# Attention and gated MLP on one core: attention scores from three products of split operands, and the steps around them put in another order

## The reference, cut to what matters

```python
B, H, S, D = 4, 8, 576, 64                      # fp32 throughout
scores = q @ k.T / 8 + bias[h, i, j]            # bias: a two-layer MLP of log distances
attn = softmax(scores)                          # row maximum subtracted, sum + 1e-9
x = (attn @ v), heads side by side              # 2304 tokens x 512
out = (sigmoid(x @ w_gate) * (x @ w_val)) @ w_out    # 512 -> 1536 -> 512
```

## Time and profile before

| | |
|---|---|
| median of three runs | 822.9 us (821.3 to 824.1) |
| the profiled execution: its own time / its span | 825.04 us / 823.2 us |
| mean granted TensorE clock over the span | 0.987 |
| busy: PE, DVE, ACT, POOL | 95%, 40%, 41%, 24% |
| bias stage | 0 to 79.2 us |
| attention stage | 79.2 to 361 us |
| MLP stage | 361 to 823 us |

### The profile page before, as it was taken

The page is one execution under the profiler, slowest core; times in us unless marked ns, Lnnn a source line. Parts: engine busy times, 40 slices in busy tenths (PEclk is TensorE's granted clock), DMA queues, the critical chain, the costliest instruction groups (busy, mean ns, idle before and its releaser), DMA issues.

```text
span 823.2 us, 13263 instructions
## 1 busy us (share of the span) xinstructions
PE 782.6 (95%) x5008; PEld 627.8 (76%) x5008; DVE 332.0 (40%) x797; ACT 338.0 (41%) x683; POOL 194.9 (24%) x362
## 2 busy tenths in 40 slices
PE   5684999999999999999989999999999999999998
PEld 2232666666666666669978998999899889989996
DVE  5894766666666666633320221123022202211220
ACT  5794666666666666643321221122022212212210
POOL 0000666646545545668400000000000000000000
PEclk9998999999999999999989999999999999999999
DMA  6684233242242233213322000100010010000001
GB/s 157 167 204 129 57 102 84 72 106 62 67 121 60 66 85 84 62 55 98 115 76 77 1 1 14 64 1 1 27 52 1 14 64 1 1 26 14 1 2 38
DMA packets 89152, 49.91 MB, mean 61 GB/s; under 512 B 60928, under 2 KB 80512, under 8 KB 89088
## 3 DMA queue, kind: packets, MB, share of 16 engines
q1 hardware_dynamic: 89088, 49.06, 21.9%
HBM read 28.98 MB, written 9.44 MB: 47 GB/s over the span
## 4 chain that ended last, share of the span: by engine, by line
PE 84%; DMA 5%; DVE 3%; ACT 3%; POOL 2%; SPq 1%; issue 1%; POOLq 0%; DVEq 0%; ACTq 0%
PE f_ps L950 18%; PE g_ps L900 15%; PE u_ps L900 15%; PE v_ps L882 10%; PE so_ps L816 9%; PE ty_ps L829 4%; PE tx_ps L841 3%; PE so_ps L811 2%; DVE feats L656 2%; DMA w_raw<-in_w_gate 2%; DMA x_raw<-in_w_out 2%; PE so_ps L764 2%; POOL w L480 1%; DMA bias<-bias_rows 1%; ACT feats L524 1%
## 5 line engine op out<-in xcount | busy, mean ns | idle before, releaser
L559 ACT ACTIVATE probs<-neg_scores,neg_max 128x576 f32<-128x576 f32 x144 | 110.6, 770 | 93.0 <-DVE neg_max L671 93.0
L900 PE MATMUL g_ps<-x_h,w 128*128 128x384 f32 x576 | 146.6, 335 | 1.2 <-DVE hid L733 1.2
L900 PE MATMUL u_ps<-x_h,w 128*128 128x384 f32 x576 | 146.3, 334 | 0.0
L733 DVE TENSOR_TENSOR hid<-u_ps,sig 128x384 f32<-128x384 f32 x72 | 40.1, 557 | 244.7 <-PE u_ps L900 244.7
L671 DVE CUSTOM_DVE_ANT_0 neg_scores<-so_ps,bias 128x576 f32<-128x576 f32 x144 | 104.0, 756 | 75.8 <-PE so_ps L816 54.6
L463 POOL TENSOR_SCALAR probs<-probs,recip 128x512 f32<-128x512 f32 x128 | 89.0, 695 | 187.6 <-DVE recip L685 187.6
L900 PEld LDWEIGHTS g_ps<-x_h,w 128*128 128x128 f32 x576 | 103.9, 188 | 2.3 <-DVE hid L733 1.6
L900 PEld LDWEIGHTS u_ps<-x_h,w 128*128 128x128 f32 x576 | 103.9, 188 | 0.5 <-issue 0.5
L620 ACT ACTIVATE h_h<-hid 128x384 fp32r<-128x384 f32 x72 | 37.9, 527 | 149.0 <-DVE hid L733 149.0
L900 PE MATMUL g_ps<-x_l,w 128*128 128x384 f32 x288 | 96.3, 334 | 0.0
L900 PE MATMUL u_ps<-x_l,w 128*128 128x384 f32 x288 | 96.2, 334 | 0.0
(11 more groups left out here) (68 smaller groups left out, 989.3 us busy)
## 6 DMA issues: line engine op xcount, KB each, us to landing
bias<-bias_rows SPq DMA_DIRECT2D x64, 144.0 KB
x_raw<-attn_transposed SPq DMA_DIRECT2D x6, 768.0 KB, 4.6
out<-out_sb SPq DMA_DIRECT2D x18, 256.0 KB, 2.0
q_raw<-in_q SPq DMA_DIRECT2D x32, 128.0 KB, 2.6
k_raw<-in_k SPq DMA_DIRECT2D x32, 128.0 KB, 2.5
v_main<-in_v SPq DMA_DIRECT2D x32, 128.0 KB, 2.3
w_raw<-in_w_gate SPq DMA_DIRECT2D x12, 256.0 KB, 2.9
w_raw<-in_w_val SPq DMA_DIRECT2D x12, 256.0 KB, 2.9
```

What stands on the lines that cost most here:

```text
L559: nc.scalar.activation(probs[s % RING][:, place, :], neg_scores[s % 2][:, place, :], ACT.Exp, bias=neg_max[:, stat(s, place)], scale=-1.0, ...
L733: nc.vector.tensor_tensor(hid[f % 2][:, :], u_ps[f % 3][:, 0:CH], sig[f % 2][:, :], ALU.mult).then_inc(gated, 1)
L900: last = nc.tensor.matmul(bank[f % 3][:, 0:CH], w[:, f, part, i, t, :], x[:, t, :], start=m == 0, stop=m == len(terms) - 1)
```

## The change

Scores are no longer fp32 products. q and k are held as a high part (float32r, written by ScalarE) and a low part (the difference, float32r, written by VectorE), and each score is the sum of three float32r products: high by high, low by high, high by low. The row tiles stay. Step 4's scores lie in the other two banks.

q is transposed two pairs ahead, in step 4 (the second pair's in the bias stage, at unit 18); k stays one pair ahead, in step 1, now ahead of the values. The values of a pair are computed wholly during the next one: three key tiles, two, three, two, in steps 0 to 3. Group 0 is copied out by VectorE, group 1 by ScalarE. In the steps with two places ScalarE does place 0's exponential behind `move_a`. There is one tile for the shifted scores instead of two. The drain holds three gate sums, one of them a step earlier.

```diff
-        EARLY_GATES = {STEPS: 0, STEPS + 1: 1}
+        EARLY_GATES = {STEPS - 1: 0, STEPS: 1, STEPS + 1: 2}
-        VALUE_SLOTS = {4: (0, 0, (0, 1)), 0: (1, 0, (2, 3)), 1: (1, 0, (4,)), 2: (1, 1, (0, 1, 2)), 3: (1, 1, (3, 4))}
+        VALUE_SLOTS = {0: (0, (0, 1, 2)), 1: (0, (3, 4)), 2: (1, (0, 1, 2)), 3: (1, (3, 4))}
...
+            def high_q(pair):
+                act.wait_ge(q_turned, pair + 1)
+                if pair >= 2:
+                    act.wait_ge(scored, SPP * (pair - 1) - 1)
+                nc.scalar.activation(qk_h[pair % 2][:, Q_MAIN:], q_turned_ps(pair), ACT.Copy).then_inc(q_high, 1)
...
-                if m == 1 and pair >= 1:
-                    copy_values(pair - 1, 0)
                 if m == 4 and pair >= 1:
-                    copy_values(pair - 1, 1)
-                for u, place in units:
+                    copy_values(pair - 1)
+                if m == 4 and pair + 2 < PAIRS:
+                    high_q(pair + 2)
+                if m == 1 and pair + 1 < PAIRS:
+                    high_k(pair + 1)
+                for u, place in units[:1]:
                     exponentials(s, u, place)
                 if 0 <= s - LAG < STEPS:
                     move_a(s - LAG)
                 if m == 0 and pair + 1 < PAIRS:
-                    copy_tails(pair + 1)
-                if m == 1 and pair + 1 < PAIRS:
-                    copy_q(pair + 1)
+                    high_tails(pair + 1)
+                for u, place in units[1:]:
+                    exponentials(s, u, place)
...
+            def low_q(pair):
+                dve.wait_ge(q_high, pair + 1)
+                nc.vector.tensor_tensor(qk_l[pair % 2][:, Q_MAIN:], q_turned_ps(pair), plain(qk_h[pair % 2][:, Q_MAIN:]),
+                                        ALU.subtract).then_inc(q_low, 1)
...
+                if m == 4 and pair + 2 < PAIRS:
+                    low_q(pair + 2)
+                if m == 1 and pair + 1 < PAIRS:
+                    low_k(pair + 1)
                 if 0 <= s - LAG < STEPS and (s - LAG) % SPP != R:
                     move_b(s - LAG)
-                if m == 1 and pair + 1 < PAIRS:
-                    copy_k(pair + 1)
+                if m == 1 and pair >= 1:
+                    copy_values(pair - 1)
+                if m == 0 and pair + 1 < PAIRS:
+                    low_tails(pair + 1)
...
             def turn_q(pair):
                 pe.wait_ge(q_in, 16 * Q_DMAS * (pair + 1))
-                if pair >= 2:
-                    pe.wait_ge(x_ready, 2 * (pair - 2) + 1)
+                if pair >= 3:
+                    pe.wait_ge(x_ready[1], pair - 2)
...
+                terms = ((high, high), (high, low), (low, high))
...
+                    for n, (qq, kk) in enumerate(terms):
...
+                        for place in (1, 0):
+                            rows = slice(place * D, (place + 1) * D)
+                            last = nc.tensor.matmul(score_ps(s, place)[:, a, :],
+                                                    qq[rows, Q_MAIN + m * P:Q_MAIN + (m + 1) * P], kk[rows, keys],
+                                                    start=n == 0, stop=n == len(terms) - 1)
...
+                if m == 1 and pair + 1 < PAIRS:
+                    turn_k(pair + 1)
+                if m == 1 and pair >= 1:
+                    values(pair - 1, *VALUE_SLOTS[m])
+                if m == 4 and pair + 2 < PAIRS:
+                    turn_q(pair + 2)
```

More of the change, by code:

```diff
@@ L31 @@
 PREP_UNIT = 6
+SECOND_UNIT = 18
 PAIRS = B * H // 2
@@ L114, in program @@
         valued = sem("valued")
-        x_ready = sem("x_ready")
+        x_ready = [sem(f"x_ready{i}") for i in range(2)]
         x_stored = [sem(f"x_stored{i}") for i in range(2)]
@@ L242, in bias_ps, with score_ps, q_turned_ps @@
             return so_ps[:, 2 * i:2 * i + 2, 0:HALF]
-        def score_ps(place):
-            return so_ps[:, 2 * place:2 * place + 2, 0:HALF]
+        def score_ps(s, place):
+            at = 2 if s % SPP == R else 2 * place
+            return so_ps[:, at:at + 2, 0:HALF]
+        def q_turned_ps(pair):
+            return tx_ps[:, 0:NT * P] if pair == 1 else v_ps[:, 0:NT * P]
         def set_rows(j):
@@ L394, in _ @@
                     load_k(pair + 2)
+                if m == 0 and 1 <= pair < PAIRS - 2:
                     sp.wait_ge(q_turned, pair + 2)
@@ L800, in scores @@
                 pair, m = divmod(s, SPP)
-                tile = qk[pair % 2]
+                high, low = qk_h[pair % 2], qk_l[pair % 2]
+                terms = ((high, high), (high, low), (low, high))
                 if m == 0:
-                    pe.wait_ge(k_copied, pair + 1)
-                    pe.wait_ge(tails_copied, pair + 1)
-                    pe.wait_ge(q_copied, pair + 1)
+                    pe.wait_ge(k_low, pair + 1)
+                    pe.wait_ge(tails_low, pair + 1)
+                    pe.wait_ge(q_low, pair + 1)
                 if s >= 1:
@@ L809, in scores @@
                     keys = slice(a * HALF, (a + 1) * HALF)
-                    if m == R:
-                        last = nc.tensor.matmul(score_ps(0)[:, a, :], tile[:, Q_TAIL:Q_MAIN], tile[:, keys],
-                                                start=True, stop=True)
-                        continue
-                    for place in (1, 0):
-                        rows = slice(place * D, (place + 1) * D)
-                        last = nc.tensor.matmul(score_ps(place)[:, a, :],
-                                                tile[rows, Q_MAIN + m * P:Q_MAIN + (m + 1) * P], tile[rows, keys],
-                                                start=True, stop=True)
+                    for n, (qq, kk) in enumerate(terms):
+                        if m == R:
+                            last = nc.tensor.matmul(score_ps(s, 0)[:, a, :], qq[:, Q_TAIL:Q_MAIN], kk[:, keys],
+                                                    start=n == 0, stop=n == len(terms) - 1)
+                            continue
+                        for place in (1, 0):
+                            rows = slice(place * D, (place + 1) * D)
+                            last = nc.tensor.matmul(score_ps(s, place)[:, a, :],
+                                                    qq[rows, Q_MAIN + m * P:Q_MAIN + (m + 1) * P], kk[rows, keys],
+                                                    start=n == 0, stop=n == len(terms) - 1)
                 last.then_inc(scored, 1)
@@ L891, in gate_part @@
                 if n == 0 and i == 0:
+                    pe.wait_ge(shifted, ALL - 1)
+                if n == 2 and i == 0:
                     pe.wait_ge(shifted, ALL)
@@ L909, in _ @@
                     turn_k(0)
+                if u == SECOND_UNIT:
+                    turn_q(1)
                 bias_unit(u)
@@ L913, in _ @@
                 pair, m = divmod(s, SPP)
-                back, group, tiles = VALUE_SLOTS[m]
-                of, c = pair - back, s - LAG
+                c = s - LAG
                 if s < STEPS:
                     scores(s)
-                if m == 1 and of >= 0:
-                    values(of, group, tiles)
+                if m == 1 and pair + 1 < PAIRS:
[4 more added lines that the diff above has]
+                    turn_q(pair + 2)
                 tails_of = pair + 1 if m == 0 and pair + 1 < PAIRS else None
@@ L927, in _ @@
                     turn_tails(tails_of)
-                if m == 1 and pair + 1 < PAIRS:
-                    turn_k(pair + 1)
-                    turn_q(pair + 1)
-                if m != 1 and of >= 0:
-                    values(of, group, tiles)
+                if m in (0, 2, 3) and pair >= 1:
+                    values(pair - 1, *VALUE_SLOTS[m])
                 if s in EARLY_GATES:
```

118 lines of the change are left out of this document (70 added, 48 removed).

## The result

| | before | after |
|---|---|---|
| median (20 runs each) | 822.0 us (820.2 to 824.1) | 825.4 us (823.8 to 829.8) |
| ratio of after to before | | 1.0047, 95% interval 1.0036 to 1.0057 |
| profiled execution: own time / span | 825.04 / 823.2 us | 825.99 / 824.2 us |

The change makes the kernel 0.5% slower. The time lies in the forecast range, 1.7 us above the forecast. The forecast gave the largest chance, 0.48, to no change that can be told; what came is a change that can just be told, and slower by over 0.3% had the chance 0.30.

A forecast was written before the change was run, and what follows sets the result against it. TensorE was taken to bound the kernel at 17.73 us a pair. Terms +1.7 + 0.6 - 1.8 - 1.1 - 0.3 + 1.7 = +0.8 on the median 822.9 gave 823.7 us, range 817 to 830.

The forecast's parts named there:

- The scores: TensorE's scores: two heads cost 1.00 us instead of 1.17, with a float32r product every 0.134; 0.85 saved a pair.
- The rival with bare loads: Row tiles' weight loads not hidden: 0.225 instead of 0.134 us a product, kernel 850 us or more; chance 0.04.
- The turn: ScalarE and VectorE from shift to shift: 3.36 us instead of 2.78, with `move_a` between the two exponentials.
- Both waits: TensorE waits 0.44 us ahead of `turn_q` in step 4 and 0.25 ahead of step 0's `transpose_b`.
- TensorE keeps the pace: Rival: TensorE alone sets a pair at 16.88 us, kernel 814.4; chance 0.22 for this or near it.
- 13 pairs: Steady attention pairs: 17.6 us a pair instead of 17.73, in all -1.8 us.
- wait for `x_half`: Step 4: TensorE's `turn_q` waits 0.44 us for ScalarE's copy of group 1.
- Pair 14: From step 1 of pair 14 to that of pair 15: 16.4 us instead of 17.5, so -1.1.
- The start: Bias stage, up to the first shift: +1.7 us, bounds 0 to 3.1.
- Unit 7: Bias stage: low parts of q, tails and k, with VectorE waiting on ScalarE's high parts, cost 1.15 us there.
- a low part of 0.69 at unit 18: Bias stage: VectorE's low part at unit 18 adds 0.69 us to the start.
- The weight line: Serial weight loads and splits behind the attention: start 10.8 us after the last step 4, +1.7; length stays 55.42.

The follow-up runs named there:

- e3: Kernel after, with VectorE's low part of q behind `move_b` in step 4 instead of ahead of it: ratio to before 1.0017, 823.3 us.
- e2: Kernel after, with both exponentials of a step ahead of `move_a` on ScalarE again: ratio to before 0.9977, 820.6 us.
- e10: Kernel e8, with `turn_q` behind `transpose_b` in step 4 on TensorE: ratio to before 0.9838, 809.3 us.
- e7: Kernel before, with the split float32r products added in its old order: ratio to before 1.0002, 822.5 us.
- e5: Kernel after, with the second pair's q handled at the bias stage's end and pair 2's q loaded in step 0 of pair 0: ratio to before 1.0026.
- e4: Kernel after, with weight loads issued ahead of the last pair's stores, two before each group: ratio to before 0.9996, 821.9 us.
- e6: Kernel after, each score one fp32 product of the high parts, low parts still made: ratio to before 1.0111, 831.3 us.
- e9: Kernel after, with two early gate sums in the drain instead of three: ratio to before 1.0042, 826.4 us.
- e11: Kernel after, with the second part of w_out split one f later: ratio to before 1.0066, 828.6 us.
- e1: Kernel after, with pair 2's q loads moved from the bias stage's store queue to step 0 of the attention: ratio to before 1.0045, 825.9 us.
- e8: Kernel after, with the edits of e2, e3, e4 and e5 together: ratio to before 0.9855, 810.1 us.

## Why the prediction was right, and where it was not

**The scores: right.** 0.98 for 1.00, and 0.133 for 0.134 from product to product. The rival with bare loads falls with it. The Trainium skill, page "TensorE: Matmul & The Clock Gate", section "The mechanism", lists overlap of a weight load with running matmuls only for another row group. Here all six products of a head have the same, and those of step 4, over the whole array, do too; both come every 0.133, so the loads stay hidden in float32r: the trace disagrees with that line. Another sentence of the same section also allows a load ahead where it goes to the background weight buffer, and that fits.

**The turn: right, to 0.1 at each mark.** Both waits stand where they were foreseen. e3 takes the second away, and e2 with e10 the first, so their causes are shown. Each handoff between engines had a row, and adding up rows from engine to engine held. TensorE's own sum was right as well: 16.88 by the rows, 16.87 in after less its waits, and 16.87 in e7. "TensorE keeps the pace" was the first rival. No run makes it quite true: e10, the nearest, has 17.02, with 0.17 of waiting left. Its ratio is 0.0209 below that of after (17 us), the edits at both ends included.

**13 pairs: -1.1 for -1.8**, a pair of 17.65 for 17.60. The term that was too small is the wait for `x_half`, 0.58 for 0.44; the other wait was 0.20 for 0.25, and the prediction's own steps and waits add up to 17.57. **Pair 14: -0.6 for -1.1.** Here the step that failed is "Pair 14 turns no q, so its two waits vanish": 16.4 was forecast and 16.88 measured, because with or without q every step still has place 0's exponential behind `move_a`. In e2, without that order, this pair takes 16.25.

**The start: mis-sized, +1.7 for +3.3,** which is outside the bounds of 0 to 3.1 too. Unit 7 cost what it should: the next features start at 22.10 instead of 21.05, though VectorE then idles another 0.80 at 27.43. The failed term is "a low part of 0.69 at unit 18". It was priced as work; it is work and a handoff, in which VectorE, which ran ahead of ScalarE, lost 2.25 of that lead. 2.25 + 0.61 is near the 2.6 that e5 brings back. The same rule stood in the sum for unit 7 (0.69 + waiting) and was left out for unit 18. How exact the 3.3 is: the seven profiled executions with this start unchanged (after, e2, e3, e4, e6, e9, e11) have the first shift at 80.55 to 82.88, mean 82.1. Against the one of before that is +2.9, still well above 1.7; before has a single profiled execution. The upper bound of 3.1 leaned on two loads in the queue at 0.6 each, 1.2 in all, for which e1 shows 0.4.

**The weight line: right in size, wrong in part in its reason.** +1.6 for +1.7, and the line's length is unchanged. Of "two gates and all five tiles of values stand ahead of the store", the five tiles stood between the last step 4 and the store in before too, so they add nothing. The second gate is worth 0.6 by e9; the rest are waits that the values used to fill.

**What the prediction did not have: the half clock behind the idle time.** It read the 3.00 at 420.32 as a sign that TensorE's work is free there, which e4 and e11 confirm, but not that the products behind it ran at half clock and cost 2.8 more, which another idle place could take from them. So the profiled pair shows +1.0 and the medians +3.4. That the forecast of +0.8 came out near the first is luck: the start's 1.6 too little and the pairs' 1.2 too much gained are together 2.8 too low, and the half clock's place gave 2.8 back.

Open: why pair 0 takes 0.8 more. e2 gives back 0.45 of it, and e7, in the old order, has 0.6 of it already. The half clock at the start of the attention lasts 13.7 in after and 10.2 in before and e7, but pair 0 takes 18.87 in after and e9, where it ends 10.5 and 9.3 after the first shift, so the clock isn't shown to set it. Open too: how VectorE came to its lead over ScalarE at unit 18, and how often the half clock falls behind the first output products, since a profile is one execution.

## What to carry to other kernels

Time saved on the busiest engine only counts up to the next chain of handoffs: lay that chain out link by link, with each in-order queue, and order the instructions so that the longest turn has nothing between its links, here 0.58 of a copy between two exponentials, worth 5.8 us. Read a wait from start to start: e6 and e10 each have one of 0.17 that lies under the last matmul and shows no idle time. Price an instruction that waits for an engine which runs behind by the lead that it gives up, not by its duration. Keep loads that start a long line of transfers ahead of stores that wait for results, and look at what runs behind idle time of TensorE, since it may run at half clock.

## What was not expected of the hardware

- After idle time of 3.0 to 6.8 on TensorE the granted clock was 0.50 for the 3.4 or 6.8 us shown, over whatever came next: 419.4 (before), 407.0 (after, 3.80 idle), 422.9 (e11, 6.80 idle). In e8, with 0.56 of idle time at that place, it stayed at 1.00. An idle place that lies beside a DMA line costs nothing twice, in the wait and in the clock; removed, both turn up where they cost (e11).
- The weight line took 55.0 to 57.6 us from its first load to the first output product in the profiled executions of the ten kernels that issue its loads in the same order, and 54.7, 56.8 and 58.1 in the three with the other order (e8, e4, e10).
- A float32r product of 288 columns in two row tiles comes every 0.133, 0.013 above its columns at 2.4 GHz, though each has its own weight load.
